# A first expert's output product taken out of the per-batch tiles and done in five phases of seven products

## The reference

```python
def _attn_ref(q, k, v, p):            # 8 batches, 8 heads, 576 tokens, head size 64, 32 packs
    p_packed = sm_attn(p, k, v)       # softmax(scale * p k^T) v
    return sm_attn(q, p_packed, p_packed)

def _moe_ref(x, w_gate, w_val, w_out, rms_g):     # 4608 tokens, 512 -> 1536 -> 512
    rms = np.sqrt(np.mean(x * x, axis=-1, keepdims=True) + 1e-06)
    xn = x / rms * rms_g
    g = xn @ w_gate
    silu = g * (1.0 / (1.0 + np.exp(-g)))
    return silu * (xn @ w_val) @ w_out            # "the first expert"

def _moe2_ref(x, w_in, w_out, alpha):             # 4608 tokens, 512 -> 2048 -> 512
    h = x @ w_in
    g = np.maximum(h, 0.0) + alpha * np.minimum(h, 0.0)
    return g @ w_out                              # "the second expert"
```

## Time and profile before

| | |
|---|---|
| runs | 1441.87, 1443.06 and 1443.10 us, median 1443.06 |
| profiled execution | 1442.03 us, its span 1440.2 us, clock 0.999 |
| PE busy | 1429.2 us (99%), 9334 matmuls |
| DVE, ACT, POOL busy | 958.0 (67%), 716.1 (50%), 316.9 (22%) us |
| DMA | 314.16 MB, 218 GB/s on average |
| start to the first block | 0 to 28 us |
| tile 0 | 28 to 122.2 us |
| tiles 1 to 6 | 122.2 to 634.1 us, 85.3 us each |
| tile 7 and the rest tile | 634.1 to 736.75 us |
| five rounds | 736.75 to 1437 us |

### The profile page before, as it was taken

One profiled execution on the slowest core, in us unless ns is written; L12 is line 12 of the kernel. 1 busy time (PEld: TensorE's weight loads), 2 busy tenths in 40 slices (PEclk: granted clock), 3 DMA queues, 4 the chain that ended last, 5 costly groups with the idle time before them and its releaser, 6 DMA issues.

```text
span 1440.2 us, 24192 instructions
## 1 busy us (share of the span) xinstructions
PE 1429.2 (99%) x9334; PEld 1230.1 (85%) x9334; DVE 958.0 (67%) x1530; ACT 716.1 (50%) x1174; POOL 316.9 (22%) x543
## 2 busy tenths in 40 slices
PE   8999999999999999999999999999999999999998
PEld 4988878888887888889888888888888888889998
DVE  6775756647575664742337885788678857886786
ACT  4454454445445444532235653565456545654564
POOL 2803545243454424443800000000000000000000
PEclk9999999999999999999999999999999999999999
DMA  9414586866868687347237867777777777768775
GB/s 359 142 42 139 157 285 187 237 224 176 271 168 265 187 235 231 98 136 246 88 116 253 287 230 237 254 278 246 230 259 279 240 241 249 256 232 261 253 265 187
DMA packets 174770, 314.16 MB, mean 218 GB/s; under 512 B 22208, under 2 KB 128704, under 8 KB 160192
## 3 DMA queue, kind: packets, MB, share of 16 engines
q1 hardware_dynamic: 174512, 312.56, 67.1%
...
q10 hardware_dynamic: 144, 0.07, 0.0%
...
## 4 chain that ended last, share of the span: by engine, by line
PE 97%; DVE 1%; ACT 0%; DMA 0%; issue 0%; SPq 0%; DVEq 0%; ACTq 0%
PE psum L924 31%; PE psum L926 30%; PE psum L925 30%; PE psum L1122 3%; PE psum L1023 1%; PE psum L947 1%; PE psum L996 1%; DMA k_sb<-k_t 0%; PE psum L1052 0%; PE psum L1051 0%; PE psum L1055 0%; PE psum L981 0%; DVE g_sb L1990 0%; PE psum L961 0%; PE psum L1087 0%
## 5 line engine op out<-in xcount | busy, mean ns | idle before, releaser
L924 PE MATMUL psum<-an_hi,m_hi 128*128 128x288 f32 x768 | 232.4, 303 | 1.2 <-DVE an_lo L1830 1.2
L925 PE MATMUL psum<-an_hi,m_lo 128*128 128x288 f32 x768 | 225.9, 294 | 0.0
L926 PE MATMUL psum<-an_lo,m_hi 128*128 128x288 f32 x768 | 225.7, 294 | 0.0
L924 PE MATMUL psum<-stage_hi,ring 128*128 128x480 f32 (+1 forms) x560 | 206.9, 369 | 0.1
L926 PE MATMUL psum<-stage_lo,ring 128*128 128x480 f32 (+1 forms) x560 | 206.8, 369 | 0.0
L925 PE MATMUL psum<-stage_hi,ring 128*128 128x480 f32 (+1 forms) x560 | 206.8, 369 | 0.0
L924 PE MATMUL psum<-x_hi,ring 128*128 128x480 f32 (+1 forms) x560 | 206.8, 369 | 0.0
L926 PE MATMUL psum<-x_lo,ring 128*128 128x480 f32 (+1 forms) x560 | 206.8, 369 | 0.0
L925 PE MATMUL psum<-x_hi,ring 128*128 128x480 f32 (+1 forms) x560 | 206.8, 369 | 0.0
L1562 ACT CAST stage_hi<-g_sb 128x480 fp32r<-128x480 f32 (+1 forms) x240 | 138.0, 578 | 121.6 <-PE psum L926 121.6
L2002 DVE TENSOR_TENSOR stage_lo<-g_sb,stage_hi 128x480 fp32r<-128x480 f32 (+1 forms) x240 | 150.1, 634 | 49.3 <-ACT stage_hi L1562 48.9
...
## 6 DMA issues: line engine op xcount, KB each, us to landing
...
k_sb<-k_t SPq DMA_DIRECT2D x16, 576.0 KB, 5.2
...
```

The source lines that it names most:

```text
L924: nc.tensor.matmul(dst, w_hi, hi, start=start, stop=False, skip_group_check=onto)
L925: nc.tensor.matmul(dst, w_lo, hi, start=False, stop=False, skip_group_check=onto)
L926: return nc.tensor.matmul(dst, w_hi, lo, start=False, stop=stop, skip_group_check=onto)
```

## The change

The output product leaves the tiles. A tile is now its 24 blocks and the attention; ACT writes the silu into six slots (`ACTS`), DVE multiplies in place, and SP stores each chunk of the hidden features to a DRAM buffer `h_mid`. From block 6 of tile 0 on, blocks alternate between two pairs of PSUM banks, 0/1 and 4/5. `an_hi` and `an_lo` are double. All six folds' weights stay in SBUF, so that their reloads (33 DMAs of 1 MB) go.

The first expert's output product becomes five phases "out", with the same 464 or 448 columns as the rounds now have, each with seven products of six units; they stand before the rounds (out 0, out 1) and between them. Their weights come from 12 further parts made by POOL, 44 in all, up to seven a tile, from tile 0 on. `normed` and `scaled` move from POOL to DVE (for c > 0); the first `tokens` now wait for `scaled` too. The scores, maxima, `exp` and `turn_keys` of batch c + 1 move a tile forward, and folds 4 and 5 into the next tile. First-round x is taken from the output buffers by DMA and prepared by ACT and DVE in out 1, no longer by POOL.

```diff
-WIDTHS = [480, 480, 480, 480, 384]
+WIDTHS = [464, 464, 464, 464, 448]
+PARTS_OF = [4, 6, 7, 7, 7, 7, 6, 0]
...
+LATER = {                                   # batch c = b + 1, 2 <= c < 8, in tile b
+    "PE": {("between", 0): ["packed"], ("within", 2): ["turn_packed"],
+           ("ready", 3): ["tokens0_ready"], ("after", 3): ["tokens0"],
+           ("within", 5): ["tokens1_ready", "tokens1"],
+           ("between", 11): ["gram0", "fold0_ready", "fold0"],
+           ("between", 14): ["gram1", "fold1_ready", "fold1"],
+           ("within", 17): ["means"], ("ready", 18): ["fold2_ready"], ("after", 18): ["fold2"],
+           ("ready", 20): ["fold3_ready"], ("after", 20): ["fold3"]},
+    "DVE": {("after", 0): ["norm0", "norm1", "packed"], ("after", 2): ["scaled"],
+            ("after", 3): ["turn_s0", "gram"], ("after", 4): ["max2_0", "shift0"],
+            ("after", 5): ["turn_s1", "max2_1"], ("within", 6): ["shift1"], ("within", 7): ["gram_lo"],
+            ("between", 7): ["sums0"], ("after", 8): ["probs0"], ("after", 9): ["turn_p0", "sums1"],
+            ("within", 10): ["probs1"], ("after", 10): ["a2_lo0", "turn_p1"], ("after", 11): ["a2_lo1"],
+            ("after", 12): ["weigh0"], ("after", 13): ["fold0"], ("after", 14): ["sum_lo0"],
+            ("after", 15): ["weigh1"], ("after", 16): ["sum_lo1", "fold1"], ("after", 17): ["means"],
+            ("after", 18): ["newton"], ("after", 19): ["normed0"], ("after", 20): ["normed1", "fold2"],
+            ("after", 21): ["split0"], ("after", 22): ["split1", "fold3"]},
+    "Activation": {("after", 2): ["packed"], ("after", 4): ["gram_hi"], ("after", 6): ["probs0", "probs1", "silu"],
+                   ("after", 10): ["a2_hi0"], ("after", 11): ["a2_hi1"], ("after", 12): ["fold0"],
+                   ("after", 14): ["sum_hi0"], ("after", 15): ["fold1"], ("after", 16): ["sum_hi1"],
+                   ("after", 18): ["rsqrt"], ("after", 19): ["fold2"], ("after", 20): ["split0"],
+                   ("after", 21): ["split1"], ("after", 22): ["fold3"]},
+}
+NEXT = {                                    # batch c + 1 in the same tile
+    "PE": {("ready", 9): ["scores0_ready"], ("after", 9): ["scores0", "scores1_ready", "scores1"]},
+    "DVE": {("between", 11): ["max0"], ("between", 13): ["max1"], ("between", 15): ["turn_keys"]},
+    "Activation": {("between", 9): ["scores0", "scores1"], ("between", 13): ["exp0", "exp1", "silu"]},
+}
+CARRIED = {                                 # batch c - 1
+    "PE": {("ready", 0): ["fold4_ready"], ("after", 0): ["fold4"], ("ready", 6): ["fold5_ready"], ("after", 6): ["fold5"]},
+    "DVE": {("after", 1): ["fold4"], ("after", 7): ["fold5"]},
+    "Activation": {("after", 1): ["fold4"], ("after", 7): ["fold5"]},
+}
...
+PHASES = [("out", 0), ("out", 1), ("up", 0), ("down", 0)]
+for t in range(1, ROUNDS):
+    PHASES += ([("out", t + 1)] if t + 1 < ROUNDS else []) + [("up", t), ("down", t)]
...
+        def pair_of_banks(n):
+            return 0 if n < SINGLE or n % 2 == 0 else 4          # SINGLE = 6
...
-                for part, dst in ((0, gate_ps), (1, val_ps)):
...
+                n = BLOCKS_OF * b + i
+                for part, dst in ((0, gate_ps(n)), (1, val_ps(n))):
+                    reached(pe, silu_done if part == 0 else h32_done, block_before(n))
...
+            def wide(k, p, ups):
+                w, depth, dst = width_of(k), DEPTH[k], pair_ps(k, p, width_of(k))   # DEPTH 6 in "out", 8 in "down"
+                pair_free(k, p, ups)
+                for begin, end in WIDE_PARTS[WIDE[k][0]]:
+                    weights = next_page()
+                    for j in range(begin, end):
+                        u = UNIT_AT[k] + depth * p + j
+                        pe.wait_ge(stage_lo_done, u + 1)
+                        for side in range(2):
+                            mm = three_passes(dst[:, side, :], weights[:, j - begin, side, 0, :], ...
```

More of the change, by code:

```diff
@@ L54 @@
-DVE_PLACES = {
-    (1, "between", 1): ["fold0"],
-    (1, "between", 2): ["weigh0", "sums1"], (1, "after", 3): ["probs1"], (1, "between", 3): ["turn_p1", "fold1"],
-    (1, "within", 4): ["a2_lo1"], (1, "after", 4): ["sum_lo0"], (1, "between", 4): ["weigh1"],
-    (1, "after", 5): ["sum_lo1"], (1, "within", 6): ["means"], (1, "between", 6): ["fold2"], (1, "between", 7): ["newton"],
-    (1, "between", 8): ["fold3"], (1, "between", 10): ["fold4"], (1, "after", 11): ["split0"],
-    (1, "between", 11): ["split1"],
-}
@@ L72 @@
+    ("after", 4): ["gram1"], ("between", 4): ["mean1"],
 }
 DVE_FIRST = {
[3 rows of a table removed]
+    ("after", 0): ["fold2"], ("after", 1): ["fold3"], ("after", 2): ["sums1"], ("between", 2): ["probs1"],
+    ("after", 3): ["turn_p1"], ("after", 4): ["weigh1"], ("within", 5): ["mean1"],
+    ("between", 7): ["newton1", "normed1"], ("within", 10): ["split1"],
 }
 ACT_FIRST = {
-    (0, "after", 0): ["fold2"], (0, "after", 1): ["fold3", "fold4", "fold5"],
-    (0, "between", 6): ["rsqrt1"], (0, "within", 9): ["split1"],
+    ("after", 0): ["fold2"], ("after", 1): ["fold3", "fold4", "fold5"],
@@ new lines @@
+    "DVE": {("between", 3): ["max0", "max1"], ("between", 5): ["turn_a0", "norm0", "norm1"],
+            ("after", 6): ["turn_a2"], ("within", 7): ["packed"], ("between", 7): ["scaled"],
+            ("within", 9): ["turn_s0", "gram"], ("after", 9): ["max2_0", "shift0"],
+            ("after", 10): ["turn_s1", "max2_1"], ("within", 11): ["shift1"], ("after", 11): ["gram_lo"],
[3 rows of a table added]
+            ("after", 19): ["sum_lo1"], ("after", 20): ["means"], ("after", 21): ["newton", "fold1"],
+            ("after", 22): ["normed0", "normed1"], ("within", 23): ["split0"], ("after", 23): ["split1", "fold2"],
+            ("between", 23): ["fold3"]},
@@ L98 @@
 }
 LATER = {
-    "PE": {(0, "between", 7): ["packed"], (0, "after", 8): ["turn_packed"],
-           (0, "ready", 9): ["tokens0_ready"], (0, "after", 9): ["tokens0"],
-           (0, "ready", 10): ["tokens1_ready"], (0, "after", 10): ["tokens1"]},
-    "DVE": {(0, "between", 2): ["max0"], (0, "after", 3): ["max1"], (0, "between", 4): ["turn_keys"],
-            (0, "between", 5): ["norm0", "norm1"], (0, "within", 8): ["packed"],
-            (0, "after", 9): ["turn_s0", "gram"], (0, "after", 10): ["shift0"], (0, "between", 10): ["turn_s1"],
-            (0, "within", 11): ["shift1"], (1, "after", 0): ["gram_lo"],
-            (1, "between", 0): ["sums0"], (1, "after", 1): ["probs0", "turn_p0"], (1, "after", 2): ["a2_lo0"]},
@@ L111 @@
+NEXT_BUT_ONE = {
+    "PE": {("ready", 13): ["scores0_ready"], ("after", 13): ["scores0"],
+           ("ready", 15): ["scores1_ready"], ("after", 15): ["scores1"]},
+    "DVE": {("between", 16): ["max0"], ("between", 17): ["max1"], ("between", 19): ["turn_keys"]},
+    "Activation": {("after", 14): ["scores0"], ("between", 15): ["scores1"], ("after", 17): ["exp0", "exp1", "silu"]},
 }
 CARRIED = {
-    "PE": {(0, "ready", 0): ["fold5_ready"], (0, "after", 0): ["fold5"]},
-    "DVE": {(0, "after", 4): ["fold5"]},
@@ L653, in block_of_y @@
[L653 to L666 removed]
+                n = PART_PLACES[b].get(i)
@@ L1952, in _ @@
             dve.wait_ge(consts_set, 4)
[L1953 to L1954 removed]
+            for name in ("max0", "max1", "norm0", "turn_a0", "turn_a2", "norm1", "packed", "turn_s0", "gram", "max2_0", "shift0",
+                         "turn_s1", "sums0", "probs0", "turn_p0", "max2_1", "weigh0", "fold0e0", "mean0", "fold0e1", "newton0",
```

1411 lines of the change are left out of this document (629 added, 782 removed), and 9 rows, old and new, of tables (DVE_FIRST, SECOND).

## The result

| | before | after |
|---|---|---|
| time, median of 4 runs each | 1442.9 us (1441.9 to 1443.1) | 1460.9 us (1458.3 to 1463.0) |
| profiled execution: time, span | 1442.0, 1440.2 us | 1460.5, 1458.7 us |
| ratio, 95% interval | | 1.0123 (1.0107 to 1.0139) |

A forecast was written before the change was run, and what follows sets the result against it. PE bounds the kernel (97% of the chain); 1442.0 - 37.6 = 1404.4, plus 0.4 + 9.5 + 20.5 + 2.0 + 7.2 + 1.5 + 1.0 gives 1446.5 us profiled, 1447.5 median; own range 1439 to 1456, outer 1413 to 1464.

The forecast's parts named there:

- the rival of the transfers: In the tiles: DMA transfers set tile length; at 60 us a tile, five tiles lose 2.5 more: 1460 us; chance 0.09.
- Signs of both: Forecast: PE waits on a_lo, sq_split, act_sb and m_lo in middle tiles; transfers: PE or PEld waits on k_sb, POOL on parts_raw.
- The product's cost: On PE: 299.9 us of matmuls leave the tiles, five out phases add 262.3 us, rounds keep 699.5: net -37.6 us.
- out 1*'s term of 1.0: In phase out 1: DVE's 55 us of work against PE's 53, taken as 1.0 us, bounds 0 and 5.
- The walk: Through a full tile: PE loses 4.1 us waiting for DVE and ACT; tiles 1 to 5 20.5 us, tile 6 2.0.
- the means: Blocks 12 to 17 of a full tile: PE wants the means' operand at 25.5 us, ready at 27.8: 2.3 us lost.
- silu: Blocks 12 to 17 of a full tile: product 14 and DVE wait for silu 14; PE's gate 16 loses 0.35 us.
- gram0: Blocks 6 to 11 of a full tile: PE wants a2_lo0 for gram0 at 12.0 us, gets it at 13.0: 1.0 lost.
- Tile 0: First tile: waits by a walk of its own order cost 9.5 us, bounds 3 and 15; length near 68 us.
- The port: DVE and POOL sharing SBUF's port: about 0.15 us on eight two-input DVE instructions, 1.2 us a tile, 7.2 in six.
- The keys' load: In the tiles: lands 4.7 us after issue, has 8 us, 4.5 in tile 0; 1.5 us in all, bounds 0 and 15.

The follow-up runs named there:

- e4: Changed kernel with POOL's forming of the weights' parts left out from the fourth part on, loads and stores kept: 1447.7 us, ratio 1.0035.
- e2: Changed kernel with another instruction order on VectorE and ScalarE in tiles 1 to 6: 1452.3 us, ratio 1.0065.
- e10: Changed kernel with e2's order, parts' transfers three blocks later, parts spread 5, 7, 6, 6, 6, 6, 7, 1, new tile 0 order: 1440.1 us, ratio 0.9981.
- e12: e10 with parts spread 5, 6, 6, 6, 6, 7, 7, 1 and tile 0's third to fifth behind blocks 21, 22, 23: 1439.6 us, ratio 0.9969.
- e5: e2's kernel with only one product of seven stored from the 13th part on, up and down phases reading other pages: 1435.9 us, ratio 0.9949.
- e11: Changed kernel with only the parts spread over the tiles as 5, 7, 6, 6, 6, 6, 7, 1: 1453.2 us, ratio 1.0066.
- e7: Changed kernel with a deliberate pause of PE ahead of the fourth product of each of the five down phases: 1482.0 us, ratio 1.0269.

## Why the prediction was right, and where it was short

The side held: the product's 37.6 us are won on PE and more than that is lost in the tiles. The time did not: 1460.9 us lies above the forecast's own range of 1439 to 1456 and next to the rival of the transfers (1460), which had a chance of 0.09. It is within 1413 to 1464 only because that range was drawn out to this rival. Signs of both were found: PE's waits name sq_split, a_lo and act_sb as forecast, and k_sb as under the rival. By the prediction's own steps:

- **The product's cost** held to 1.1 us (962.9 against 961.8), and *out 1*'s term of 1.0 was not needed as such: DVE has 47.9 us in it and not the 55 I had counted, and PE ran through it without a wait.
- **The walk** of a full tile was right in place and too large. With the port it took 4.1 + 1.2 = 5.3 us a tile. In tiles 1 to 5 PE's waits for DVE and ACT come to 11.7 us, 2.3 a tile: the means 1.7 to 1.8 each where 2.3 were taken, silu up to 0.6 where it was 0.35, gram0 0.7 and 0.3 in two tiles and none in the others where it was 1.0 in each. Tiles 1 and 2 are 5.9 and 5.2 us above 52.2, of which 1.7 each is the clock (0.03 of their length). With POOL idle (e4) the excess is 3.3 and 3.9 at full clock. e2 shows that the means' wait is a matter of order, as reordering took it from 10.6 to 3.5 us.
- **Tile 0** was put near 68 us and took 73.9. The clock is at 0.82 in the stretch from 90 to 100 us. DVE stood for 4.2 us in front of product 21 while the inverse root was ready; e10 and e12 took 4.5 to 6 us out of the tile by order.
- **The port** had 7.2 us (1.2 a tile). An instruction loses 0.13 to 0.19 us where 0.15 was taken, so the mechanism and its price are the ones named. More instructions lose it than the eight that were counted: DVE's time rises by some 2 us a tile (41.4 to 43.5). What of this reaches the time is not shown; e4's 12.7 us hold SP's waits and the clock as well, and in tiles 1 and 2 the stretches, less the clock, are 0.9 us longer and 0.4 shorter than with POOL idle.
- **The keys' load** is a term that failed: 1.5 us taken in all, 9.4 us of waits found. The step is "it lands 4.7 us after issue and has 8 us". It landed in 6.1 us in the median, and above all in tiles 3 to 5 it was issued 4 to 7 us later behind the tile's start than in e5 (15.3 to 18.2 us and not 11.4), as SP takes up to 4.6 us for an issue ahead of it. The rival of the transfers had priced this, 2.5 us in each of five tiles, by volume; e5 shows that it is real (16.7 us with e2's order), e11 that spreading gives 8.2.
- **The clock** was in no term, and that without a reason. The losses (1 - clock) x length of the seven tiles are 15.5 us, an upper bound, as in part of that time PE stood still anyway. 9.1 of them are in tiles 3 to 5, where each slow stretch stands behind a wait for the keys; tile 1's stands behind the end of tile 0 and tile 2's behind the means. e7 shows the mechanism alone.

In sums: the profiled time is 14.0 us above the sum of 1446.5. The tiles took 462.4 us (28.9 to 491.3) where PE needs 408.9 (28.0 to 736.75 before, less 299.9), so 53.5 of waiting and clock where the terms gave 9.5 + 20.5 + 2.0 + 7.2 + 1.5 = 40.7: 12.8 short. Tiles 1 to 5 have 6.6 of it (295.6 us against 5 x (52.2 + 4.1 + 1.2) + 1.5 = 289.0), tiles 0, 6 and 7 the rest. The first tile began at 28.9 and not at 28.0, where 0.4 was taken. In tiles 1 to 5 the excess over 5 x 52.2 is 34.6 us: at most 12.5 of clock, 9.1 of waits for the keys, and some 13 for walk and port together where 26.5 were forecast. So part of the sum's closeness is luck: a walk that was some twice too large stood in for a clock and a transfer that were left out. These are differences of stretches, in which port, keys and clock are contained together, and not separate measurements.

What stays open: how the port and SP's waits for POOL divide e4's 12.7 us, whether bytes or packets make SP's issues long, and why the slow stretch of the clock is 3 to 5 us long.
